# Wider placeholder products in the first attention stage, and three low parts of weights made on GpSimd

## The reference

```python
scores = scale * np.matmul(q_c, k_full.transpose(0, 1, 3, 2))   # per chunk
a = softmax(scores); out[:, :, c_start:c_end] = np.matmul(a, v_full)
x = out.transpose(0, 2, 1, 3).reshape(B * S, H * D)             # 3072 x 512
x = (1 / (1 + np.exp(-(x @ w_gate)))) * (x @ w_val) @ w_out     # d_ff 1536
h = x @ w_in                                                    # d_ff 2048
P = a[0] + a[1]*h + a[2]*h**2 + a[3]*h**3
Q = 1.0 + abs(b[0])*abs(h) + abs(b[1])*h**2
y = (P / (Q + 1e-6)) @ w_out2
```

## Time and profile before

| What | us |
|---|---|
| Median of 3 runs | 1165.22 |
| Lowest and highest | 1165.10, 1166.02 |
| The profiled execution's own time | 1163.57 |
| Its span, first to last instruction | 1161.6 |
| PE busy in the span | 1145.8 (99%) |
| DVE busy | 926.5 (80%) |
| ACT busy | 750.9 (65%) |
| POOL busy | 123.3 (11%) |

### The profile page before, as it was taken

One profiled execution on the slowest core, in us unless ns is written; L12 is line 12 of the kernel. 1 busy time (PEld: TensorE's weight loads), 2 busy tenths in 40 slices (PEclk: granted clock), 3 DMA queues, 4 the chain that ended last, 5 costly groups with the idle time before them and its releaser, 6 DMA issues.

```text
span 1161.6 us, 20825 instructions
## 1 busy us (share of the span) xinstructions
PE 1145.8 (99%) x7954; PEld 942.8 (81%) x7954; DVE 926.5 (80%) x1419; ACT 750.9 (65%) x1224; POOL 123.3 (11%) x150
## 2 busy tenths in 40 slices
PE   7899999999999999999999999999999999999998
PEld 6788887778888777888888888888888888888887
DVE  5886767776676777777667998988988988988987
ACT  3665555455555555555556877877877877877875
POOL 2052230012233001223100000000000000000000
PEclk9999999999999999999999999999999999999999
DMA  7511412742141374323137100200200200200100
GB/s 261 165 64 55 163 55 95 230 149 91 60 157 55 100 234 158 109 86 105 46 129 264 42 1 1 73 1 1 72 0 0 72 0 0 72 0 0 37 1 37
DMA packets 40720, 94.05 MB, mean 81 GB/s; under 512 B 4288, under 2 KB 4288, under 8 KB 40640
## 3 DMA queue, kind: packets, MB, share of 16 engines
q1 hardware_dynamic: 40640, 92.95, 23.7%
HBM read 80.35 MB, written 12.58 MB: 80 GB/s over the span
## 4 chain that ended last, share of the span: by engine, by line
PE 94%; DVE 3%; issue 1%; DMA 1%; ACT 0%; SPq 0%; POOL 0%; ACTq 0%; POOLq 0%; DVEq 0%
PE ps_h L1253 9%; PE ps_h L1255 9%; PE ps_h L1260 9%; PE ps_h L1417 7%; PE ps_h L1412 7%; PE ps_h L1413 7%; PE ps_y L1456 7%; PE ps_y L1452 7%; PE ps_y L1450 7%; PE ps_y L1332 5%; PE ps_y L1337 5%; PE ps_y L1333 4%; PE ps_h L1235 2%; PE ps_h L1211 2%; PE ps_y L1321 1%
## 5 line engine op out<-in xcount | busy, mean ns | idle before, releaser
L1253 PE MATMUL ps_h<-xop,wop 128*128 128x512 f32 x484 | 188.3, 389 | 0.0
L1255 PE MATMUL ps_h<-xop,wop 128*128 128x512 f32 x484 | 188.3, 389 | 0.0
L1412 PE MATMUL ps_h<-x_split,weights 128*128 128x512 f32 x384 | 149.4, 389 | 0.0
L1413 PE MATMUL ps_h<-x_split,weights 128*128 128x512 f32 x384 | 149.4, 389 | 0.0
L1260 PE MATMUL ps_h<-xop,wop 128*128 128x512 f32 x484 | 149.0, 389 | 0.0
L1450 PE MATMUL ps_y<-weights,hid 128*128 128x512 f32 x360 | 140.0, 389 | 0.0
L1452 PE MATMUL ps_y<-weights,hid 128*128 128x512 f32 x360 | 140.0, 389 | 0.0
L878 DVE TENSOR_TENSOR wop<-rawp,wop 128x448 fp32r<-128x448 f32 x144 | 91.1, 661 | 32.7 <-ACT wop L494 32.7
L757 ACT ACTIVATE tmp<-ps_h 128x512 f32<-128x512 f32 x96 | 57.2, 595 | 92.4 <-PE ps_h L1417 92.4
L899 DVE TENSOR_TENSOR x_raw<-ps_h,probs_t 128x512 f32<-128x512 f32 x70 | 48.1, 687 | 79.6 <-PE ps_h L1260 79.3
L1332 PE MATMUL ps_y<-hid,wout 128*128 128x512 f32 x264 | 105.7, 400 | 0.6 <-DVE stage_h L930 0.3
(11 more groups left out here) (103 smaller groups left out, 2277.9 us busy)
## 6 DMA issues: line engine op xcount, KB each, us to landing
rawp<-wgv_l SPq DMA_DIRECT2D x36, 512.0 KB, 3.8
oraw<-wo_l SPq DMA_DIRECT2D x72, 256.0 KB, 3.9
unit<-v_l SPq DMA_DIRECT2D x24, 512.0 KB, 4.5
unit<-k_l SPq DMA_DIRECT2D x24, 368.0 KB, 4.2
unit<-q_l SPq DMA_DIRECT2D x24, 256.0 KB, 3.4
x_stage<-y_dram SPq DMA_DIRECT2D x6, 1024.0 KB, 5.7
out<-stage SPq DMA_DIRECT2D x24, 256.0 KB, 2.3
braw<-wb_l SPq DMA_DIRECT2D x11, 512.0 KB, 5.6
```

What stands on the lines that cost most here:

```text
L1253: nc.tensor.matmul(dst, w_h[k], xop[:, m, 0, k, :], start=first and k == 0, stop=False, skip_group_check=True)
L1255: nc.tensor.matmul(dst, w_l[k], xop[:, m, 0, k, :], start=False, stop=False, skip_group_check=True)
L1412: nc.tensor.matmul(dst, lhs(c, 0), x_split[:, 0, c, :], start=(c == 0), stop=False)
L1413: nc.tensor.matmul(dst, lhs(c, 1), x_split[:, 0, c, :], start=False, stop=False)
```

## The change

Two things change, both in the first round alone.

First, the placeholder products. `WARM` goes from 3 to 6 and the opening call from `2 * WARM` to `WARM`, so the first six products stay as they are. Every other group of three products of 128 columns becomes one product of the identity by 512 columns of zeros (`wide_fill`), with a new buffer `zeros` that POOL sets to zero at the start. The buffer lies in the memory of `hid1`, which is written only after the first round's attention. In the first pair the single product at place 0 is dropped and the single product at place 1 becomes one of 512 columns.

Second, pieces 1 to 3 (of 0 to 3) of the low part of chain 1's weights are made by POOL, each once ACT has made the high part, and not by DVE. POOL does this between the quarter sums of chain 1 and those of chain 2. DVE waits for `w_lo >= 8` before the first low part of chain 2.

```diff
-WARM = 3
+WARM = 6
+        zeros = at("zeros", 155648, [P, 512])
@@ gpsimd
+            nc.gpsimd.memset(zeros[:], 0.0).then_inc(ident_done, 1)
-            for c in range(CHAINS * NS):
+            weight_sums(0)
+            weight_sums(1)
+            for i in range(1, 4):
+                cols = slice(448 * i, 448 * (i + 1))
+                pool.wait_ge(w_hi, 5 + i)
+                pool.wait_ge(w_lo, 4 + i)
+                nc.gpsimd.tensor_tensor(wop[:, 1, 1, cols], rawp[:, 1, 256 + 448 * i:256 + 448 * (i + 1)],
+                                        wop[:, 1, 0, cols].bitcast(F32), ALU.subtract).then_inc(w_lo, 1)
+            for c in range(2, CHAINS * NS):
                 weight_sums(c)
@@ vector, split_w
+                if c == 2 and i == 0:
+                    dve.wait_ge(w_lo, 8)
@@ vector, last_operands
-                if s == 0:
-                    split_w(1, 3)
@@ vector, at_start
                 elif (p, place) == (3, 1):
-                    split_w(1, 1)
                     token_sum(0, T1, 0)
                     token_sum(0, T2, 0)
-                elif (p, place) == (3, 2):
-                    split_w(1, 2)
@@ tensor
+            def wide_fill():
+                nc.tensor.matmul(ps_y[:, 3, :], ident[:], zeros[:], start=True, stop=True)
                     if b == 1:
-                        warm_up(WARM)
+                        pe.wait_ge(ident_done, 3)
+                        wide_fill()
@@ tensor, fill_first
                 elif (p, place) == (4, 1):
-                    warm_up(WARM)
+                    wide_fill()
                     early_product(1, M2)
-                elif place != 2:
-                    warm_up(1 if p == 0 and place < 2 else WARM)
+                elif place != 2 and (p, place) != (0, 0):
+                    wide_fill()
-            warm_up(2 * WARM)
+            warm_up(WARM)
```

## The result

The changed kernel took 1168.53 us (median of 14 runs, 1163.37 to 1172.40), the kernel before 1165.23 us (median of 14). The ratio is 1.0028, 95% interval 1.0017 to 1.0040: slower, by about 3.3 us, where 1163.3 us and a gain had been forecast. The time also lies above the range given, 1161.2 to 1167.0. Single runs of one kernel differ by some us here (those of the changed kernel by up to 9), so medians and intervals decide and one profile only shows where things stand. The profiled execution of the changed kernel took 1167.53 us, its span 1165.7.

What follows compares the result with a forecast made beforehand. PE bounds the kernel, paced by instruction arrival in the first attention stage; -2.09 (records) + 0.3 (fills) - 0.17 (DVE) = -1.96, taken as -1.9, gave 1163.3 us; own range 1162.0 to 1164.6, over all cases 1161.2 to 1167.0.

Steps and rivals of the forecast that it cites:

- Blocks of 127 records: First round's attention: PE runs dry of instructions every 127 records, making six gaps, 6.08 us in all.
- The seventh boundary of before: First attention stage: boundary before the last 30 scores records moves 58 records on, 18 into the next weighing.
- the blocks arrive at the same times as before: First attention stage: the block of 43.04 us still comes then and finds PE further on, at the point of 45.13.
- the 2.09 us of gain: First attention stage: fewer records, with block arrivals unchanged, let PE gain 45.13 - 43.04 = 2.09 us.
- Rival 1: First attention stage: gaps stay as long, 1.9 us of longer fills stand on PE; +1.7 us, 1166.9, chance 0.18.
- the eighth boundary: Last weighing: boundary moves from its start to near its end, a further 1.1 us gap, 1168.0.
- The Trainium skill on block crossings: Instruction refills: crossings mostly hidden, so fewer instructions worth nothing; the prediction held this untrue in the first attention stage.
- The fills' length: First attention stage: each wide fill takes 0.2 us longer, 1.9 us of PE time, of which 0.3 stays.
- the rivals with the half clock gone (2 and 3): 2: fills pass through, half clock gone, +0.3, 1165.5, chance 0.12; 3: blocks set pace, clock gone, -3.1, 1162.1, chance 0.20.
- The low parts on POOL: Chain 1: moving three low parts off DVE gains 0.17 us; POOL's cost of 0.5 us is covered by slack.
- Rival 4, the early load: Last weighing: chain 3's earlier 512 KB load delays its instruction block by 1.1 us; -0.8 us, 1164.4, chance 0.08.

Runs made afterwards that it cites:

- e2: The changed kernel with the low parts back on DVE, so only the wide fills against the kernel before; ratio 1.0030.
- e7: The kernel before with the first attention stage's fills left out, except the one between the first two scores; ratio 1.0060.
- e4: The kernel before with each group of three fill products streaming 512 columns in all (128, 192, 192), instruction stream unchanged; ratio 1.0002.
- e6: The kernel before with the wide fills alone, plus 31 tiny products (62 records) in early PE waits; ratio 1.0006.
- e3: As e2, but each wide fill is one product of 384 columns instead of 512; ratio 1.0041 to the kernel before.
- e1: The kernel before with the three low parts of chain 1 on POOL, fills unchanged; ratio 1.0001.
- e9: The changed kernel plus 31 tiny products (62 records) in early PE waits; ratio 0.9992 to the kernel before.
- e11: The changed kernel plus 40 tiny products in early PE waits; ratio 1.0008 to the kernel before.
- e5: The kernel before plus 33 tiny products (66 records) in PE's waits at 7 and 9 us, no wide fill; ratio 1.0057.
- e8: The kernel before with the low parts on POOL, plus 16 tiny products (32 records) in PE's waits at 7 and 9 us; ratio 1.0047.
- e12: The changed kernel plus 48 tiny products in early PE waits; ratio 1.0040 to the kernel before.

## Why the prediction was wrong, point by point

*Blocks of 127 records, and that they make the gaps: right.* The seventh boundary of before, with 30 records left in scores, was said to move to 18 records into the weighing behind. In e2 the gap that ends at 48.30 us leaves 46 of the 64 records of that weighing: 18 had gone by.

```profile
48.30 0.90 PE L1237 MATMUL ps_h<-probs_t,unit 64*64 64x32 f32 x46 [1.40 <-issue]
```

*That the blocks arrive at the same times as before: wrong, and this is the step that failed.* From it came the 2.09 us of gain. The release at 43.04 us was to stay and find PE 58 records further on. In fact the releases moved with the program: they came 5.75 us apart, not 4.9. The seven packets of before start at 11.21, 16.72, 22.76, 26.53, 31.44, 35.33 and 40.79 us, those of after at 10.53, 15.95, 21.62, 27.26, 33.07, 39.10 and 44.99: the first three earlier, the others later, the seventh by 4.2 us. The seventh is under way in these two answers, for 40.75 to 40.85 us of before and for 44.95 to 45.05 us of after:

```profile
q8 instruction: 1, 0.02, 54.8%
```
```profile
q8 instruction: 1, 0.02, 54.9%
```

The record at which PE was to be at 43.04 us, 18 into a weighing, it reached some 4 us later, in this row of after (46.78 + 18/64 x 1.40 = 47.2), part of the way at half clock. Before, the same record was reached at 45.13: the 2.0 us by which the stage ends later are all there.

```profile
46.78 1.40 PE L1243 MATMUL ps_h<-probs_t,unit 64*64 64x32 f32 x64
```

At every boundary with a gap of 0.4 us or more in the first stage, in before and all versions but e7 (which has none), PE goes on 2.2 to 2.6 us after its packet started, but for four; in those it took up to 3.4 us, and the packet itself took 1.3 to 2.0 us. A gap is this time, less that of the records which PE still has in front of the boundary: the packet of 15.95 us found PE with work up to 17.45, and PE went on at 18.39, so 2.44 - 1.50 = 0.94. Fewer instructions are fewer boundaries, but half a block fewer in eight is none in the stage. What the change did was to move the boundaries against the packets: before, the packet for the boundary near 29 us started 86 records ahead of it, and that boundary cost nothing; after, the five in a row had 63 down to 27 records, and each cost 0.94 us or more.

*Rival 1 is the one that happened, in its sign, and with its price near (1166.9, or 1168.0 with the eighth boundary).* I gave it 0.18. Its mechanism was named half: the gaps did stay, 5.9 us of them from 10 us on against 6.1, with longer fills beside them. But it put the loss on the fills' length, and e4 and e6 show that the length costs 0.8 and 0.2 us of stage in one profile each and nothing that the timing can tell, while e3, without it, is as slow as the change. That its number came near is not shown to be more than luck. The extra gap in the last weighing was not seen.

*The Trainium skill on block crossings.* Runtime: NRT & Kernel Launch, section Instruction fetch mechanics, has them mostly hidden. In the first stage the traces show up to 2.86 us at one of them. In the long stretches of products of 512 columns no gap put down to "issue" is seen (PE is busy 1095.47 of 1100.40 us behind the stage), and there the page and the trace agree.

*The fills' length: right.* 1.02 and 1.12 us against 0.83 and 0.94, so 0.19 more; 0.2 was taken.

*The clock: the rivals with the half clock gone (2 and 3) fell.* The half clock came in the changed kernel too, from 42.07 to 45.50 us, while e2 had none from 13 to 64 us (the table of busy time, after first, then e2; the clock is the third number from the end) and was as slow:

```profile
42.07:45.50 3.43, 3.43 (x73) 1.73 (x69) 2.44 (x4) 1.06 (x2) 1.17 (x1) 0.50 0.53 171
```
```profile
13.00:64.00 51.00, 41.57 (x934) 27.66 (x932) 39.93 (x71) 27.05 (x47) 5.68 (x7) 1.00 0.50 163
```

So it does not decide. That fuller fills spare it is not shown; that leaving them out brings it on is (e7).

*The low parts on POOL: not contradicted in sum, wrong in their prices.* -0.17 us was forecast; 1.0001 was measured, with an interval of some 1.8 us either way, which can't tell it from nothing. A POOL instruction took 1.13 to 1.17 us, not 1.3 to 2.1 (448/256 of 0.7 would have been 1.2), and it stretched one DVE operation by 0.93 us (e1), where at most 0.54 had been allowed.

*Rival 4, the early load, did not come true in the changed kernel:* its packets of 44.99 and 50.92 us took 0.88 us each, and the last weighing has no gap. In e1, e9 and e11, which have the early load too, the packet that starts between 44.2 and 46.3 us took 1.9 to 2.1 us; in e11 a gap of 2.04 us follows at 49.65. Whether the load did that was not tested.

*What was not counted.* That the change moves every later instruction of PE against the blocks, and so makes gaps in the third round, 1.1 us, hundreds of us behind the last edited line. e2 and e3 have such gaps as well, e4, e6 and e9 have none, and e5 shows the same gap from tiny products alone. How the rest of the later 2.08 us splits is open: between single profiles this stretch varies by more (1100.3 in e9, 1102.4 in e4 without any such gap, 1103.9 in e1, where a load of v was waited for).

## What to carry to other kernels

Where PE runs many small products, count its instructions between the gaps that the profile puts down to "issue". If the count is constant and a packet on the instruction queue goes ahead of each gap, they are block boundaries, and any edit that adds or removes PE instructions moves all later ones: compare it with a version padded to the same count before crediting or blaming the edit. The same test turned a loss of 0.28% into a tie here, without touching the work.

## What the runs showed of the hardware that was not expected

- 33 tiny products (66 records) put into idle time made the kernel before 0.57% slower (e5), 6 to 7 us.
- At the five gaps after the change, PE went on 2.2 to 2.4 us after the block's packet started, though such a packet of 16 KB took only 0.92 to 0.96 us.
- The five longest gaps at boundaries (2.40 to 2.86 us, one each in e5, e8, e9, e11 and e12) stand where the packet started only when PE had nothing of its block left to start.
- A stage at half clock for 41 us (e7) ended only 5 us later than before, with no gap of more than 0.24 us inside a group.
- A DVE operation of 0.69 us took 1.62 us beside a POOL operation of 1.13 us (e1).
